# A state recurrence and two feed-forward blocks on one core: far keys of the second chunk on partitions 64 to 127, 48-column update weights, and turns and updates gathered in one unit each

## The reference

```python
for t in range(S):                      # S = 768, D = 48
    cur = einsum('bhd,bhe->bhde', u * k[t], v[t])
    y[t] = einsum('bhd,bhde->bhe', r[t], state + cur)
    state = w[t][..., None] * state + einsum('bhd,bhe->bhde', k[t], v[t])
x = y.transpose(0, 2, 1, 3).reshape(3072, 384)
xn = x / sqrt(mean(x * x) + 1e-6) * rms_g
x = (silu(xn @ w_gate) * (xn @ w_val)) @ w_out          # 384 -> 1536 -> 384
h = maximum(x @ w_in, 0)
out = (s * h * h + b) @ w_out2                           # 384 -> 2048 -> 384
```

## Time and profile before

| | |
|---|---|
| Median of 3 executions | 1012.98 us |
| Profiled execution | 1013.42 us |
| its span | 1011.3 us, 24572 instructions |
| PE busy | 994.9 us (98%) |
| DVE, ACT, POOL busy | 537.8, 323.6, 268.5 us |
| Attention of stage 0 | about 6 to 60 us |
| Stages 1 to 5 beside the first feed-forward block | about 60 to 612 us |
| Second feed-forward block | about 612 to 1011 us |

### The profile page before, as it was taken

The page is one execution under the profiler, slowest core; times in us unless marked ns, Lnnn a source line. Parts: engine busy times, 40 slices in busy tenths (PEclk is TensorE's granted clock), DMA queues, the critical chain, the costliest instruction groups (busy, mean ns, idle before and its releaser), DMA issues.

```text
span 1011.3 us, 24572 instructions
## 1 busy us (share of the span) xinstructions
PE 994.9 (98%) x10584; PEld 862.9 (85%) x10584; DVE 537.8 (53%) x723; ACT 323.6 (32%) x550; POOL 268.5 (27%) x189
## 2 busy tenths in 40 slices
PE   7889999999999999999999999999999999999998
PEld 6878888888888888888888888998998989989898
DVE  6799857764676577557743225506226054161440
ACT  1442323233222313231323445406235053161340
POOL 4655723552463166216700650000000000000000
PEclk7799999999999999999999999999999999999999
DMA  7380252116013501440126201010010010100000
GB/s 273 118 327 5 90 165 93 49 51 217 33 49 111 188 3 52 155 141 3 48 61 232 69 16 64 9 39 16 16 48 0 23 39 8 54 0 16 16 8 23
DMA packets 41980, 73.99 MB, mean 73 GB/s; under 512 B 19105, under 2 KB 26273, under 8 KB 40609
## 3 DMA queue, kind: packets, MB, share of 16 engines
q1 hardware_dynamic: 41312, 71.52, 20.9%
q10 hardware_dynamic: 576, 1.13, 0.3%
HBM read 59.27 MB, written 13.37 MB: 72 GB/s over the span
## 4 chain that ended last, share of the span: by engine, by line
PE 87%; DVE 1%; issue 0%; ACT 0%; DVEq 0%
PE value_o_ps L609 13%; PE mix_gate_ps L609 13%; PE o_ps L1404 10%; PE level_ps L47 10%; PE o_ps L621 9%; PE mix_gate_ps L1404 5%; PE value_o_ps L1404 5%; PE mix_gate_ps L47 5%; PE value_o_ps L47 5%; PE value_o_ps L621 4%; PE level_ps L481 4%; PE mix_gate_ps L557 2%; PE level_ps L557 2%; PE level_ps L535 1%; PE level_ps L499 0%; PE level_ps L519 0%
## 5 line engine op out<-in xcount | busy, mean ns | idle before, releaser
L1478 DVE SCALAR_TENSOR_TENSOR sqr<-relu,sb_col 128x512 f32<-128x512 f32 x96 | 72.3, 753 | 216.9 <-ACT relu L1436 216.9
L1189 POOL TENSOR_TENSOR R<-R,arena 128x512 f32<-128x512 f32 x72 | 117.5, 1649 | 187.2 <-PE level_ps L481 161.9
L1057 DVE TENSOR_TENSOR u_raw<-value_o_ps,u_raw 128x512 f32<-128x512 f32 x66 | 45.5, 689 | 110.8 <-PE value_o_ps L609 110.8
L806 ACT ACTIVATE u_raw<-mix_gate_ps 128x512 f32<-128x512 f32 x72 | 43.1, 598 | 182.8 <-PE mix_gate_ps L609 182.7
L813 ACT ACTIVATE u_hi<-u_raw 128x512 fp32r<-128x512 f32 x66 | 41.7, 631 | 152.3 <-DVE u_raw L1057 152.3
L609 PE MATMUL value_o_ps<-x_hi,w_hi 128*128 128x512 f32 x216 | 85.1, 394 | 0.0
L609 PE MATMUL mix_gate_ps<-x_hi,w_hi 128*128 128x512 f32 x216 | 84.7, 392 | 0.0
L609 PE MATMUL value_o_ps<-x_hi,w_lo 128*128 128x512 f32 x216 | 84.1, 389 | 0.0
L609 PE MATMUL mix_gate_ps<-x_hi,w_lo 128*128 128x512 f32 x216 | 84.1, 389 | 0.0
L609 PE MATMUL mix_gate_ps<-x_lo,w_hi 128*128 128x512 f32 x216 | 84.1, 389 | 0.0
L609 PE MATMUL value_o_ps<-x_lo,w_hi 128*128 128x512 f32 x216 | 84.1, 389 | 0.0
(11 more groups left out here) (190 smaller groups left out, 2309.4 us busy)
## 6 DMA issues: line engine op xcount, KB each, us to landing
kr_nat<-kr SPq DMA_DIRECT2D x10, 1152.0 KB, 5.7
K<-kT SPq DMA_DIRECT2D x12, 512.0 KB, 4.5
arena<-wT SPq DMA_DIRECT2D x12, 512.0 KB, 6.4
R<-rT SPq DMA_DIRECT2D x10, 512.0 KB, 4.2
w_raw<-wgv SPq DMA_DIRECT2D x12, 384.0 KB, 5.2
v_sb<-v SPq DMA_DIRECT2D x12, 384.0 KB, 4.1
x_scratch<-x_sb SPq DMA_DIRECT2D x18, 256.0 KB, 2.3
x_raw<-x_scratch SPq DMA_DIRECT2D x6, 768.0 KB, 4.3
```

Of the source, the lines that this page charges most:

```text
L1057: dve.tensor_tensor(u[:, f % 2], value_ps[:], u[:, f % 2], ALU.mult).then_inc(u_done, 1)
L1189: pool.tensor_tensor(q, q, decay(blk, l, 0), ALU.mult).then_inc(rmul_done, 1)
L1478: dve.scalar_tensor_tensor(out=sq[f % 2][:], in0=relu[f % 2][:], scalar=sb_col[:, 0:1], in1=relu[f % 2][:], op0=ALU.mult, op1=ALU.mult).th ...
```

## The change

1. `far` becomes `arena[:, :, Q*P : Q*P + Q*SUB]` on all 128 partitions: chunk 0 stays on partitions 0 to 63, chunk 1 on 64 to 127. `place_far` copies both with one ACT instruction.
2. The values that meet chunk 1's `far` keys must lie on the same partitions. A new function, `values_for_far`, copies the first 64 tokens' values of chunk 1 to partitions 64 to 127 of `arena` (`v_far`), one ACT instruction per block, at unit 13 of each stage.
3. In `attend` both `far` matmuls of a head stand in step 0, the second on T(64, 64). Step 1 has none.
4. `update` takes 48 columns of weights and writes 48 partitions; the state's matmuls read 48 rows.
5. The turn of chunk 3 of a stage moves from unit 22 to 20, and the updates of chunks 2 and 3, with their `advance_state`, from 24 to 22.

```diff
-    far = arena[0:SUB, :, Q * P:2 * Q * P].rearrange("p b (c j t) -> p b c j t", c=C, t=SUB)
+    far = arena[:, :, Q * P:Q * P + Q * SUB].rearrange("p b (j t) -> p b j t", t=SUB)
+    v_far = [arena[:, blk, Q * P + Q * SUB:Q * P + Q * SUB + DM] for blk in range(2)]
...
-                    mm = pe.matmul(sums_ps(s, n)[h * SUB:(h + 1) * SUB, p * D:(p + 1) * D],
-                                   KTr[n][:, p * P + h * SUB:p * P + (h + 1) * SUB], v_sb[blk][:, c, head * D:(head + 1) * D],
+                    mm = pe.matmul(sums_ps(s, n)[h * SUB:h * SUB + D, p * D:(p + 1) * D],
+                                   KTr[n][:, p * P + h * SUB:p * P + h * SUB + D], v_sb[blk][:, c, head * D:(head + 1) * D],
...
-                q, rows = c * NP + p, slice(h * SUB, (h + 1) * SUB)
+                q, rows = c * NP + p, slice(h * SUB, h * SUB + D)
...
-                return add(c, 1, head, far[:, blk, c, h * NP + p], v_sb[blk][0:SUB, c, head * D:(head + 1) * D])
+                cols = slice(head * D, (head + 1) * D)
+                values = v_sb[blk][0:SUB, 0, cols] if c == 0 else v_far[blk][SUB:P, cols]
+                return add(c, 1, head, far[c * SUB:(c + 1) * SUB, blk, h * NP + p], values)
...
-                        mm = from_far(low, p, h)
+                        if step == 0:
+                            mm = from_far(0, p, h)
+                            mm = from_far(1, p, h)
...
                 turn_keys(s, 2)
+                turn_keys(s, 3)
             if k == 22:
-                turn_keys(s, 3)
                 update(s, 0)
                 update(s, 1)
-            if k == 24:
                 update(s, 2)
                 update(s, 3)
+            if k == 24:
                 attend(s, 0)
...
+        def values_for_far(s, blk):
+
+            wait(act, v_in[blk], (s + 1) * 16)
+            wait(act, wb_done, level_no(s, 3, blk))
+            wait(act, kmul_done, level_no(s, 3, blk))
+            wait(act, rmul_done, level_no(s, 3, blk))
+            act.activation(v_far[blk][SUB:P], v_sb[blk][0:SUB, 1], ACT.Copy).then_inc(vfar_done, 1)
...
+            if k == 13:
+                values_for_far(s, 0)
+                values_for_far(s, 1)
...
             if k == 22:
                 advance_state(s, 0)
                 advance_state(s, 1)
-            if k == 24:
                 advance_state(s, 2)
                 advance_state(s, 3)
+            if k == 24:
```

More of the change, by code:

```diff
@@ L121, in copied, with far_copied @@
     return 2 * (blk + 1) if s == 0 else 2 * (s + 2)
+def far_copied(s, blk):
+    return blk + 1 if s == 0 else s + 2
 def by_quadrant(ap, n):
@@ L274, in attention_and_gated_phase @@
     gate_done, value_done, out_done = sem("gate_done"), sem("value_done"), sem("out_done")
+    vfar_done = sem("vfar_done")
     near_done, far_done, kt_out, sq_done = sem("near_done"), sem("far_done"), sem("kt_out"), sem("sq_done")
@@ L511, in turn_keys @@
             elif s == 0 and n == 3:
-                wait(pe, far_done, copied(0, 0))
+                wait(pe, far_done, far_copied(0, 0))
             elif n == 3:
@@ L515, in turn_keys @@
             elif s > 0:
-                wait(pe, far_done, copied(s, 1))
+                wait(pe, far_done, far_copied(s, 1))
             for p in range(NP):
@@ L529, in update @@
                 wait(pe, kt_out, turned(CH * s + n + 1) + (1 if n == 0 else 0))
-            wait(pe, far_done, copied(s, 0))
+            wait(pe, far_done, far_copied(s, 0))
             pe.wait_ge(v_in[blk], (s + 1) * 16)
@@ L551, in attend @@
             wait(pe, own_placed, 2 * (s - 1) + blk + 1)
-            wait(pe, far_done, copied(s, blk))
+            wait(pe, far_done, far_copied(s, blk))
+            wait(pe, vfar_done, 2 * s + blk + 1)
             pe.wait_ge(v_in[blk], (s + 1) * 16)
@@ L595, in first_turn @@
             wait(pe, norm_done, chunks[-1] + 1)
-            wait(pe, far_done, copied(0, 1))
+            wait(pe, far_done, far_copied(0, 1))
             for k in range(KT):
@@ L740, in place_far @@
                 wait(act, level_done, matched(s, LV - 1, 1))
[L741 to L744, removed]
+                src = pairs_ps(s, 0).rearrange("p (h b j) t -> p h b (j t)", h=2, b=2)
+                dst = far.rearrange("p b (h j) t -> p h b (j t)", h=2)
+                act.activation(dst, src, ACT.Copy).then_inc(far_done, 1)
             else:
@@ L748, in place_far @@
                     wait(act, level_done, matched(s, LV - 1, blk))
[L749 to L752, removed]
+                    src = pairs_ps(s, blk).rearrange("p (h b j) t -> p h b (j t)", h=2, b=2)
+                    dst = far[:, blk].rearrange("p (h j) t -> p h (j t)", h=2)
+                    act.activation(dst, src[:, :, blk], ACT.Copy).then_inc(far_done, 1)
+        def values_for_far(s, blk):
[4 more added lines that the diff above has]
+            act.activation(v_far[blk][SUB:P], v_sb[blk][0:SUB, 1], ACT.Copy).then_inc(vfar_done, 1)
         def keys_out(s, n):
@@ L846, in attention @@
                 keys_out(s, 2)
-            if k == 22:
                 keys_out(s, 3)
@@ L861, in first_attention @@
             place_near(0, [0])
+            values_for_far(0, 0)
             place_far(0, [0])
@@ L865, in first_attention @@
             keys_out(0, 1)
+            values_for_far(0, 1)
             place_far(0, [1])
```

## The result

The changed kernel is slower. Four executions took 1020.84 us (median, 1020.55 to 1021.53), the kernel before beside them 1013.12 us. The ratio is 1.0077, with a 95% interval from 1.0059 to 1.0094. The forecast was 1022.0 us, with a range from 1019.2 to 1024.8. The profiled execution has a span of 1018.9 us, 7.6 us more than before.

What follows compares the result with a forecast made beforehand. PE's stream was taken to bound the kernel. The terms 9.3 + 0.5 - 1.25 - 0.5 + 0.6 = +8.65 us gave 1021.6 us against the median's 1012.98, stated as 1022.0 us, range 1019.2 to 1024.8 us.

Steps and rivals of the forecast that it cites:

- The bound: Whole kernel: PE, busy 994.9 of 1011.3 us, sets the end; its stream's length moves the end one to one.
- The quarter as the unit: Attention output on PE: each small matmul costs 58 ns on its own quarter; a step lasts as long as its fullest quarter.
- The first rival (the half): Attention output: half the array is the unit, saving 0.47 us a block; 1006.7 us in all; chance 0.06.
- the second (no cost in the same quarter): Rival, attention output: both matmuls of T(64, 64) overlap, leaving only small terms, -1.15 us; 1012.3 us; chance 0.05.
- +9.3 us in ten blocks: Attention output, stages 1 to 5: 16 more rounds on T(64, 64) in step 0 cost 0.93 us a block.
- Stage 0, +0.5 us: Stage 0: about 0.9 us later at PE's transposes, up to 1.2 us returned if the clock holds; ends -0.4 and +1.9.
- 48 columns, -1.25 us: State updates: 48 instead of 64 weight columns save 12 ns a round over 13 x 8 rounds; range 0 to -2.2 us.
- One unit, -0.5 us: Turns and updates gathered, stages 2 to 5: fewer shape changes on PE save 0.12 us a stage; range -0.9 to 0.
- wait at the fourth turn, +0.6 us: PE waits for ACT's copy of the first turn's bank: 0.1 us in stage 3, 0.5 in stage 4; range 0.3 to 1.1.
- The fourth rival: Stages 1 to 5: fourth-turn wait drags on a DVE or POOL step; 1024 to 1025 us; chance within forecast's shared 0.87.
- ACT, DVE, DMA: 0: Copies, state advances and loads on the other engines and queues cost 0, as PE does not wait for them.
- The sum: Whole kernel: 9.3 + 0.5 - 1.25 - 0.5 + 0.6 = +8.65 us, giving a forecast of 1022.0 us.

## Why the prediction was right, step by step

**The bound.** PE's stream set the end, before and after. Right.

**The quarter as the unit.** Right, and shown from three sides: taking 16 of 24 rounds a step from a quarter that is no fuller than two others changes nothing, taking 16 of 40 from the fullest one gives back all of the loss, and starts on T(64, 64) keep 58 ns whatever the other quarters do. The first rival (the half) and the second (no cost in the same quarter) are refuted. All of it is seen on fp32 matmuls of 64 by 64 weights and 48 moving columns; what makes the 58 ns within a quarter is not shown.

**+9.3 us in ten blocks.** Measured 9.0. In a block of two states the 16 rounds are there: T(64, 64) goes from 1.38 to 2.31 us from its first start to its last, 0.93 us. But the way from the step's last matmul on T(64, 64) to the next step's first start is 0.28 us instead of 0.32. That gives back 0.04 us a block. Before, T(0, 64) still started a matmul behind it, at 327.62 us, and now it is the last; that this is the reason is not shown.

**Stage 0, +0.5 us.** Measured -0.2 us in the profiled pair, within the ends of -0.4 and +1.9 but with the other sign. Both parts of its reasoning are seen, and both are smaller than I took. The transposes come 0.3 us later and not 0.9. In the changed kernel, against the earlier trace rows:

```profile
53.80 1.16 PE L651 MATMUL mix_gate_ps<-eye 128*128 128x128 f32 x8
56.53 0.66 PE L611 MATMUL o_ps<-eye,y 128*128 128x128 f32 x4 [1.57 <-DVE y L1034]
59.82 0.47 PE L621 MATMUL mix_gate_ps<-x_hi,w_hi 128*128 128x512 f32 x1 [0.73 <-DVE x_lo L1040]
```

```profile
54.87 0.95 DVE L1064 TENSOR_TENSOR w_lo<-w_raw,w_hi 128x768 fp32r<-128x768 f32 x1
55.74 0.74 DVE L1034 TENSOR_SCALAR y<-y,roots 128x384 f32<-128x384 f32 x2
```

The attention output ends 1.0 us later (53.80 against 52.79), not 1.5. It grew by the two blocks as I had said, but the kernel before had a stop of PE in it that I had left out of the account, and the changed kernel has none:

```profile
52.31 0.20 PE L557 MATMUL level_ps<-state,R 64*64 64x48 f32 x1 [0.41 <-issue]
```

This MATMUL starts 0.63 us behind the last one, where 0.06 us would be usual. Five more traces stop at the same place in PE's stream, from one start to the next for 0.8 to 1.4 us; none of them has both far matmuls in step 0. What PE waits for there the profile does not show. DVE's split starts 1.0 us later too, its wait of 0.59 us on POOL is gone, and so 0.35 us are left at the normalisation.

The second part is the clock, by windows (as the earlier trace rows):

```profile
52.80:56.20 3.40, 2.16 (x52) 1.85 (x48) 2.54 (x6) 2.09 (x8) 1.32 (x5) 1.00 0.37 106
56.20:60.00 3.80, 2.60 (x19) 2.21 (x20) 3.02 (x9) 2.48 (x7) 1.42 (x2) 1.00 1.00 370
```

It did not fall, after a wait of 1.57 us instead of 2.24. From the first transpose to the first feed-forward matmul the changed kernel takes 59.82 - 56.53 = 3.29 us and the kernel before 60.06 - 56.19 = 3.87, so this gives back 0.6 us. I had allowed up to 1.2, but at full clock PE waits 0.73 us for DVE there. All traces bear it out: the four without a fall take 3.3 us for this stretch, the six with one 3.8 to 4.1.

Whether the longer attention output keeps the clock up is open. Both traces with it kept the clock, but so did two of the eight without it, and in the run with the columns alone the clock fell after the same wait of 1.6 us. The sign of the term was therefore in part luck. The forecast did not hang on it: with the 0.5 to 0.8 us of a fall the changed kernel would still be inside the range.

**48 columns, -1.25 us.** Right in place, a little small (1.4 us in the run with the columns alone): (1.78 - 1.42) / 8 rounds between a run of 64 and one of 48 update MATMULs is 45 ns a round, 13.5 less than before where I took 12. The estimate of 13.3 ns by the Trainium skill's rule of columns ("TensorE: Matmul & The Clock Gate", LDWEIGHTS) is closer. The four updates of stage 3 on PE, one run instead of two of the earlier trace rows:

```profile
315.32 1.65 PE L542 MATMUL level_ps<-v_sb,arena 128*48 128x48 f32 x64
```

**One unit, -0.5 us; wait at the fourth turn, +0.6 us.** In stage 2 the whole of updates and units is -0.46 us and columns alone -0.30, so the unit gives -0.16 us where I had -0.12. The wait in stage 4:

```profile
407.38 0.60 PE L526 MATMUL level_ps<-eye,K 128*128 128x128 f32 x4
408.37 0.41 PE L526 MATMUL mix_gate_ps<-eye,K 128*128 128x128 f32 x2 [0.39 <-ACT arena L777]
```

From 407.38 + 4 x 0.11 to 408.37 us are 0.55 us without a start; the insertion as a whole grew by 0.58 us beyond the four added matmuls. The 0.39 us in brackets count from the end of the matmul ahead. In stage 3 it is 0.14 us, together 0.7 us. Stage 1 has 0.58 us as well; with the far part undone it sums to what it did before (22.22 us), since the wait on DVE's state behind it takes in what comes. Right. The fourth rival, more waiting in stages 1 to 5, is not seen.

**ACT, DVE, DMA: 0.** Right. The two value copies take 0.51 us each, the one far copy 1.01 us, and nobody waits for them.

**The sum.** The forecast had 9.3 + 0.5 - 1.15 = +8.65 us. Measured between the profiled executions are 9.0 - 0.2 - 1.1 = +7.7 us, of which their spans show 7.6. The 1 us between the two is 0.3 us of the blocks and 0.7 us of stage 0.

## What to carry to other kernels

Where small matmuls run in quarters of the array, count them per quarter and step, and look for the fullest: moving a matmul to another quarter of equal shape can cost all of its time or none, and no busy share shows it, since PE reads 98% in both cases. In this kernel the matmuls of a quarter that was no fuller than the others were free; 16 MATMULs more on the fullest quarter cost 0.89 to 0.92 us. Such a count holds between two points at which PE waits for all quarters, here one step.

An instruction moved to another unit takes a place in a queue of each engine that serves it. Look at what stands ahead of it there and what that waits for: a copy of 0.6 us cost 2.9 us of PE and then 1.6 us more by the fall of its clock, since it was put behind an instruction that waited for DVE.

## What was not expected of the hardware

- Quarters run ahead of each other in program order only a little. T(64, 0), idle in the first part of a step, began its state matmuls about three rounds before the others' `near` matmuls were through (the earlier trace rows against the first `near` at 318.68 us in the earlier trace rows), not at the start of the step. In the changed kernel T(0, 0) and T(0, 64) likewise stay bound to the pace of T(64, 64).
- Here 48 rows of weights instead of 64 change nothing (58 ns a round), 48 columns instead of 64 give 45 instead of 58.5 ns, in quarters of the same width.
- With the same work in stages 1 to 5, whose PE time repeats to hundredths, executions of one kernel differ by up to 4 us (1011.8 to 1016.1 us for the kernel before). In the ten traces of all versions stage 0 takes 58.3 to 60.9 us. The granted clock falls there in six of them, at 53.7 to 57.7 us, which costs 0.5 to 0.8 us; the rest of that spread comes earlier, since the attention output begins anywhere from 44.4 to 46.5 us and PE stops in it for up to 1.4 us at one place in six traces. What makes up the 4 us is not shown.
